# One core, attention recurrence, routing and experts: scans swapped, sat and m2 moved ahead, gate logits summed once from a table

## The chip, the cores and the metric

The kernel runs on one core of one Trainium2 chip. The metric is device time in microseconds (us), the median of the runs; lower is better.

## The reference

What is computed, cut to what matters:

```python
# r, k, v, w, a, b: [4, 8, 768, 40] float32
for t in range(768):                      # per batch and head, state is 40 x 40
    y[:, :, t] = einsum('bhd,bhde->bhe', rt, state)
    Sa = einsum('bhde,bhe->bhd', state, at)
    state = state * wt[:, :, None, :] - einsum('bhd,bhe->bhde', Sa, bt) + einsum('bhd,bhe->bhde', vt, kt)
x = y.transpose(0, 2, 1, 3).reshape(3072, 320)
# one expert of 8 per token: argmax and softmax of x @ w_gate
#   out[token] = gate * (relu(x @ w1[e]) @ w2[e])        w1 320 x 1024, w2 1024 x 320
# then a dense block: h = out @ w_in (320 x 2048); (max(h, 0) + alpha * min(h, 0)) @ w_out
```

## The kernel before

The program has three stages, one after the other: `attention` (with the routing at its end), `stage5_experts` and `stage6_dense`. The change is in `attention` alone.

`attention` cuts the 768 positions into 12 chunks of 64 and does 24 steps (`STEPS`), 16 of the 32 pairs of batch and head in each. Inside a chunk the recurrence is written as matrix products, so that only the 40 x 40 state goes from step to step. It has two passes over the steps.

**First pass**, 24 steps with no state in it. VectorE makes, for step j, the running products of the decay `w`: `suffixes(j)` scans backward (L437), `prefix_starts(j)` takes a reciprocal of the total (L442), `prefixes(j)` scans forward from it (L446). Then come two products of 512 columns, `scaled_second` (L453) and `scaled_alpha` (L456). TensorE multiplies these (`g1`, `bt`), ScalarE copies the results out of PSUM, and SyncE (SP) stores them to DRAM as blocks. The blocks are inverted on GpSimd (L118 to L127, eight steps on VectorE, L145 and L147) while the passes run on.

**Second pass**, the loop at L932 on TensorE, with a loop of its own on every other engine, 24 steps. All products of a step go through the helper `heads` (L784: 16 matmuls a product, which the trace counts as 32), in a fixed order, with a wait (`arrive`) ahead of each that needs a result of VectorE or ScalarE. Four double banks of PSUM are reused inside a step:

- BA: `alpha_s` and `g2_v` (done `w`), `low_part` (done `z`), `sat`, `m2`
- BB: `s`, then `m1` and in the end the sum that is done as `y`
- BC: `u`, `sa`, and `g2` of the next step
- BD: `ktm`, then the new state (done `st`), then `picks` (L846), which turns the rows of `yt` of the step before and multiplies them by the gate weights.

So `picks` waits for VectorE to have read the new state (`out_of["st"]`, the instruction that writes `swt` at L550), and the product that ends as `y` waits for VectorE's `m2` (L484, written from `m2_product`). VectorE does in this order in step k: `yt` of the step before (L461), its gate logits (`gates_of`, L466, read from PSUM), `alpha` for the next step (L456), the backward scan for the step after (L437), `m1` (L484), the reciprocal (L442), the sum into `w_tm` (L531), `second` (L453), the forward scan (L446), a copy of one column (L450), `swt` (L550), `m2` and `g2` (L484). ScalarE copies the products out of PSUM: `w_tm`, `st`, `ktm`, `sa_tm`, then `sa_tm` again (L758), `sat` (L760), the next inverse (L724) and the finished rows `picked` (L740). SP issues the loads, in order: the two halves of `wq` crossed between partitions (`cross_wq`), `t_in` three steps ahead, the store of `picked`, `vtm`, `vt`, an inverse, `rr`.

In the slots that are free in the last two steps VectorE does the first part of the routing (`choices_top`, L473 to L475, and `choices_one`, L479 and L480) for the 21 tiles of tokens whose logits are there by then. The last three tiles are done after the loop.

```python
                heads(from_b(lambda i, q, m: sa_tm[rows(m), slot(q ^ m, i), :]), BD, DIM, opens=False, done="st")
                arrive(out_of["sat"], i)
                heads(m2_product, BA, C, done="m2")
                arrive(s_second, i + (STEPS + 1))
                heads(with_alpha(second), BC, C, done="g2")
                arrive(out_of["st"], i + 1)
                picks()
                arrive(out_of["m2"], i)
                heads(from_b(lambda i, q, m: m2[rows(m), slot(q, i), :]), BB, C, opens=False, done="y")
```

## Time and profile before

| what | value |
| --- | --- |
| median of 3 runs | 1057.15 us (1055.74 to 1058.28) |
| profiled execution, its own time | 1054.7 us |
| its span, first to last instruction | 1052.9 us |
| TensorE matmul busy | 952.9 us (90%) |
| VectorE busy | 711.5 us (68%) |
| ScalarE busy | 442.8 us (42%) |
| GpSimd busy | 268.6 us (26%) |
| mean granted TensorE clock | 0.982 of full speed |

The span is what lies between the first and the last instruction of one execution; 1.8 us of its time lie around it. Busy shares are averages over stages that differ: the first pass runs from 0 to 139 us, the second from 139 to 373 us, the routing to 394 us, and the two expert stages fill the rest. PE is TensorE, PEld its weight loads, DVE VectorE, ACT ScalarE, POOL GpSimd, and a q behind a name is that engine's DMA queue.

### The profile page before, as it was taken

To read this page: it belongs to the slowest core of one execution; us is meant where nothing else is said; L and a number is where in the kernel's file an instruction comes from. 1 tells how busy PE (TensorE), PEld (TensorE's weight loads), DVE (VectorE), ACT (ScalarE), POOL (GpSimd) and SP (SyncE) were. 2 spreads that over 40 slices of the span, in tenths; PEclk is the share of its full clock that TensorE was granted. 3 is DMA by queue.
4 is the path that set the end of the run, shared out by engine and by line. 5 is a ranking of instruction groups with operands and counts; after the bars stand their busy time and mean duration, and the time that the engine had idled before them with its cause. 6 is when DMAs were issued, how large, how long until landed. Compare 5 with 4: busy or idle time off the path is not lost. (4 is left out here: it accounts for less than half of the span.)

```text
span 1052.9 us, 48691 instructions
## 1 busy us (share of the span) xinstructions
PE 952.9 (90%) x21425; PEld 874.8 (83%) x21425; DVE 711.5 (68%) x1076; ACT 442.8 (42%) x940; POOL 268.6 (26%) x348
## 2 busy tenths in 40 slices
PE   3526779999999998999999999879999999999997
PEld 2426769999999958998999999668999999999997
DVE  8997958899988764555555555567666565656664
ACT  5525635755555604545555555513222212222211
POOL 1009989798900003222111100241001000000000
PEclk9999988999999999999999999999999999999999
DMA  7968866898898539998676755120100101010100
GB/s 220 234 173 189 203 140 188 242 246 236 238 243 241 150 119 307 332 294 278 190 249 214 228 169 169 41 79 13 38 1 26 26 1 26 2 26 1 26 1 26
DMA packets 116866, 153.19 MB, mean 145 GB/s; under 512 B 68516, under 2 KB 87860, under 8 KB 116420
## 3 DMA queue, kind: packets, MB, share of 16 engines
q1 hardware_dynamic: 102468, 118.68, 40.3%
q0 software_dynamic: 5872, 25.28, 7.8%
q10 hardware_dynamic: 8464, 8.43, 2.4%
q8 instruction: 36, 0.59, 0.2%
q14 instruction: 26, 0.21, 0.1%
HBM read 126.72 MB, written 19.23 MB: 139 GB/s over the span
## 5 line engine op out<-in xcount | busy, mean ns | idle before, releaser
L1468 ACT CAST g_hi<-g 128x512 fp32r<-128x512 f32 x96 | 59.5, 620 | 278.0 <-DVE g L1412 274.4
L1321 PE MATMUL y_bank<-w_out_hi,g_hi 128*128 128x320 f32 x380 | 119.0, 313 | 5.1 <-DVE g_lo L1386 4.3
L1109 PE MATMUL h_bank<-xt,w 128*128 128x128 f32 x992 | 122.0, 282 | 1.8 <-issue 1.8
L1149 DVE TENSOR_TENSOR w_lo<-w_all,w_hi 128x640 fp32r<-128x640 f32 x124 | 101.7, 826 | 31.9 <-ACT w_hi L1189 27.0
L1109 PEld LDWEIGHTS h_bank<-xt,w 128*128 128x128 f32 x992 | 115.8, 195 | 6.0 <-issue 2.2
L1321 PE MATMUL y_bank<-w_out_hi,g_lo 128*128 128x320 f32 x380 | 118.0, 310 | 0.0
L1321 PE MATMUL y_bank<-w_out_lo,g_hi 128*128 128x320 f32 x380 | 117.9, 310 | 0.0
L1408 DVE TENSOR_SCALAR neg<-h_bank,slope 128x512 f32<-128x512 f32 x96 | 72.0, 750 | 65.8 <-PE h_bank L1308 65.4
L1308 PE MATMUL h_bank<-xt_hi,w_in_hi 128*128 128x512 f32 x288 | 113.1, 393 | 0.5 <-DVE xt_hi L1369 0.5
L1308 PE MATMUL h_bank<-xt_hi,w_in_lo 128*128 128x512 f32 x288 | 112.1, 389 | 0.0
L1386 DVE TENSOR_TENSOR g_lo<-g,g_hi 128x512 fp32r<-128x512 f32 x96 | 66.5, 693 | 65.9 <-ACT g_hi L1468 64.5
L1142 DVE SCALAR_TENSOR_TENSOR ht_lo<-h_bank,ht_hi 128x512 fp32r<-128x512 f32 x62 | 42.8, 692 | 88.6 <-ACT ht_hi L1182 83.7
L1189 ACT CAST w_hi<-w_all 128x640 fp32r x124 | 89.7, 727 | 29.3 <-PE y_bank L1121 20.6
L127 POOL TENSOR_TENSOR solved<-solved,share 128x31 f32<-128x31 f32 (+15 forms) x124 | 99.2, 800 | 9.7
L784 PE MATMUL bank<-alpha,second 40*64 40x64 f32 x1568 | 44.6, 269 | 56.5 <-DVE alpha L456 55.7
L124 POOL TENSOR_TENSOR share<-solved,blk 128x31 f32<-128x31 f32 (+15 forms) x124 | 89.0, 718 | 9.7
L784 PEld LDWEIGHTS bank<-alpha,second 40*64 40x64 f32 x1568 | 38.6, 178 | 59.8 <-issue 59.8
L95 POOL DMA_INDIRECT x<-x_rows_mid,order x31 | 32.1, 1035 | 197.8 <-DVE order L609 97.5
L1321 PEld LDWEIGHTS y_bank<-w_out_hi,g_hi 128*128 128x128 f32 x380 | 71.9, 189 | 10.6 <-DVE g_lo L1386 5.9
L1121 PE MATMUL y_bank<-w_hi,ht_hi 128*128 128x320 f32 x248 | 79.2, 319 | 0.0
L1182 ACT ACTIVATE ht_hi<-h_bank 128x512 fp32r<-128x512 f32 x62 | 37.1, 598 | 97.3 <-PE h_bank L1109 97.3
L1121 PE MATMUL y_bank<-w_lo,ht_hi 128*128 128x320 f32 x248 | 76.7, 309 | 0.0
(213 smaller groups left out, 2145.1 us busy)
## 6 DMA issues: line engine op xcount, KB each, us to landing
w<-w_in SPq DMA_DIRECT2D x31, 1024.0 KB
t_in<-wak_in SPq DMA_DIRECT2D x24, 679.0 KB, 5.7
t_in<-wab_in SPq DMA_DIRECT2D x21, 679.0 KB, 5.0
w_all<-w_in POOLq DMA_DIRECT2D x8, 1280.0 KB, 9.2
rr<-rr_in SPq DMA_DIRECT2D x24, 336.0 KB, 3.5
w_rest<-w_in SPq DMA_DIRECT2D x62, 128.0 KB
vtm<-vtm_in SPq DMA_DIRECT2D x24, 240.0 KB, 3.7
vt<-vt_in SPq DMA_DIRECT2D x24, 224.0 KB, 4.0
```

What stands on the lines that cost most here:

```text
L124: link(eng.tensor_tensor(part, q[:, 0:j + 1, j:j + 1].to_broadcast(shape), h[:, j:j + 1, j + 1:B].to_broadcast(shape), ALU.mult))
L127: link(eng.tensor_tensor(rest, rest, part, ALU.subtract))
L784: last = pe.matmul(out[HALF * to:HALF * to + rows_out, row, n * i:n * i + n], lhs, rhs, start=opens and i == 0, stop=closes and i == HP - 1)
L1109: last = pe.matmul(h_bank[s][h][:, f * ET:(f + 1) * ET], w1[s][:, k, (FH * h + f) * PARTS:(FH * h + f + 1) * PARTS], xt[s][:, k, :], start ...
L1121: last = pe.matmul(y_bank[s][:, 0:FEAT], h[s][:, f, :], w[:, f, :], start=f == 0 and n == 0, stop=f == NF - 1 and n == 2)
L1149: dve.tensor_tensor(piece(w2_lo, p), of_expert(e, p), piece(w2_hi, p).bitcast(F32), ALU.subtract).then_inc(s_w2lo, 1)
L1189: act.copy(piece(w2_hi, p), of_expert(e, p)).then_inc(s_w2hi, 1)
L1308: last = pe.matmul(h_bank[j % 2][:, :], w[:, k, f * PARTS:(f + 1) * PARTS], x_part[b % 2][:, k, :], start=n == 0, stop=n == len(passes) - 1)
L1321: last = pe.matmul(y_bank[n][:, 0:FEAT], g_part[j % RING][:, n * PARTS:(n + 1) * PARTS], v[:, f, :], start=f == 0 and p == 0, stop=f == NF ...
L1386: dve.tensor_tensor(g_lo[j % RING][:, :], g[j % 2][:, :], g_hi[j % RING][:, :].bitcast(F32), ALU.subtract).then_inc(s_glo, 1)
L1408: dve.tensor_scalar(neg[j % 2][:, :], h_bank[j % 2][:, :], 0.0, keep.slope[:, f:f + 1], ALU.min, ALU.mult).then_inc(s_neg, 1)
L1468: act.copy(g_hi[j % RING][:, :], g[j % 2][:, :]).then_inc(s_ghi, 1)
```

## The change

VectorE's two scans change places in both passes. The forward scan `prefixes` now comes first, the reciprocal (`suffix_starts`) is taken from its end, and the backward scan `suffixes` second. In the first pass `alpha` now comes ahead of `second`. The total decay that `swt` is multiplied by is now column C of the step's own `wq`, so the copy at L450 goes. SP's `cross_wq` waits for the forward scan of its step and, from its third call on, for the `yt` of two steps before (earlier: three steps before).

On TensorE `sat` now stands ahead of `sa`, and `m2` ahead of the product that ends as `st`. ScalarE copies `sat` ahead of `sa_tm`, and VectorE writes `m2` ahead of `swt`.

VectorE's reduce in each step of the second pass (`gates_of(k)`, 64 columns of PSUM to 8) goes. In its place ScalarE copies the 64 columns of a step into a table `gate_parts`, in memory of the first expert weights that is not in use yet, ahead of its copy of `picked`. VectorE sums 21 steps of the table in one reduce in the slot of step k = 22, ahead of `choices_top`, and the last three in one after the loop. TensorE's `ktm` waits for ScalarE's `picked` in place of VectorE's reduce.

```diff
+        gate_parts = keep.w1[0][:, :, :].rearrange("q n f -> q (n f)")[:, 0:STEPS * 2 * QP * EXPERTS].rearrange("q (k n) -> q k n", k=STEPS)
...
             def load_t(j):
                 if j >= TR:
-                    if j - TR < STEPS:
-                        sp.wait_ge(s_alpha1, j - TR + 1)
-                    elif j - TR == STEPS:
-                        sp.wait_ge(s_alpha0, 1)
-                    else:
-                        sp.wait_ge(s_second, j - TR + 1)
+                    sp.wait_ge(s_second, j - TR + 1)
...
             def cross_wq(k):
-                sp.wait_ge(s_wc, k + 1)
-                if k >= 3:
-                    sp.wait_ge(out_of["y"], k - 1)
+                sp.wait_ge(s_wq, STEPS + k + 1)
+                if k >= 2:
+                    sp.wait_ge(out_of["y"], k)
...
             def store_rows(k):
-                sp.wait_ge(s_rows, k + 1)
+                sp.wait_ge(s_rows, k + 3)
...
+            def prefixes(j):
+                dve.wait_ge(s_t[j % TR], 16 * (j // TR + 1))
+                if j >= 1:
+                    dve.wait_ge(s_suf, j)
+                dve.tensor_tensor_scan(out=forward(wq[j % 3][:, :, :]), data0=forward(w_of(j)), data1=forward(restart[:, :, :]), initial=0.0,
+                                       op0=ALU.mult, op1=ALU.add).then_inc(s_wq, 1)
+
+            def suffix_starts(j):
+                dve.wait_ge(s_wq, j + 1)
+                dve.reciprocal(restart[:, :, WIDE - 1:WIDE], wq[j % 3][:, :, C:C + 1]).then_inc(s_rw, 1)
+
             def suffixes(j):
-                dve.wait_ge(s_t[j % TR], 16 * (j // TR + 1))
+                dve.wait_ge(s_rw, j + 1)
                 if j >= 2:
                     dve.wait_ge(s_second, j - 1)
...
-            def prefix_starts(j):
+            def scaled_second(j):
                 dve.wait_ge(s_suf, j + 1)
-                dve.reciprocal(restart[:, :, 0:1], suf[j % 2][:, :, 1:2]).then_inc(s_rw, 1)
...
-            def prefixes(j):
-                dve.wait_ge(s_rw, j + 1)
...
-                dve.wait_ge(s_wq, j + 1)
-                if j >= STEPS:
-                    dve.tensor_copy(wq[j % 3][:, :, WIDE - 1:WIDE], suf[j % 2][:, :, 1:2]).then_inc(s_wc, 1)
...
-            def scaled_second(j):
...
-            def scaled_alpha(j, sem):
-                dve.tensor_tensor(alpha[:, :, :], in_of(j, 0), wq[j % 3][:, :, 0:C], ALU.mult).then_inc(sem, 1)
+            def scaled_alpha(j):
+                return dve.tensor_tensor(alpha[:, :, :], in_of(j, 0), wq[j % 3][:, :, 0:C], ALU.mult)
...
-            def gates_of(k):
-                dve.wait_ge(s_rows, k + 1)
-                gates = BD[:, :, 0:QP * PICK].rearrange("q h (p e) -> q e h p", e=PICK)[:, DIM:PICK]
-                dve.tensor_reduce(logit[:, k, :], gates, mybir.AxisListType.XY, ALU.add).then_inc(out_of["pick"], 1)
+            def gates_of(steps):
+                return dve.tensor_reduce(logit[:, steps, :], gate_parts[:, steps, :].rearrange("q k (x e) -> q k e x", e=EXPERTS), AX, ALU.add)
...
             for k in range(STEPS):
+                prefixes(k)
+                suffix_starts(k)
                 suffixes(k)
-                prefix_starts(k)
-                prefixes(k)
                 if k >= 1:
                     dve.wait_ge(did["bt"], k)
+                scaled_alpha(k)
                 scaled_second(k)
-                scaled_alpha(k, s_alpha1)
...
+            prefixes(STEPS)
+            suffix_starts(STEPS)
             suffixes(STEPS)
-            prefix_starts(STEPS)
-            prefixes(STEPS)
             dve.wait_ge(did["bt"], STEPS)
+            scaled_alpha(STEPS).then_inc(s_alpha0, 1)
             scaled_second(STEPS)
...
-            suffixes(STEPS + 1)
+            prefixes(STEPS + 1)
+            suffix_starts(STEPS + 1)
...
-            prefix_starts(STEPS + 1)
-            prefixes(STEPS + 1)
+            suffixes(STEPS + 1)
...
-                    if k >= 2:
-                        gates_of(k - 2)
-                    else:
-                        dve.sem_inc(out_of["pick"], 1)
                 dve.wait_ge(did["w"], k + 1)
                 if more:
-                    scaled_alpha(STEPS + k + 1, s_alpha)
+                    scaled_alpha(STEPS + k + 1).then_inc(s_alpha, 1)
                 if k + 2 < STEPS:
-                    suffixes(STEPS + k + 2)
+                    if k >= 1:
+                        dve.wait_ge(out_of["y"], k + 1)
+                    prefixes(STEPS + k + 2)
                 dve.wait_ge(did["m1"], k + 1)
                 masked(m1, BB).then_inc(out_of["m1"], 1)
                 if k + 2 < STEPS:
-                    prefix_starts(STEPS + k + 2)
+                    suffix_starts(STEPS + k + 2)
...
                 if k + 2 < STEPS:
-                    prefixes(STEPS + k + 2)
+                    suffixes(STEPS + k + 2)
                 elif k + 2 == STEPS:
                     dve.wait_ge(s_iota, 8)
+                    dve.wait_ge(s_gates, NTT - LATE)
+                    first_choices(gates_of(FIRST))
                     choices_top(FIRST, first_choices)
                 else:
                     dve.memset(one_hot[:, :, FINAL], 0.0)
                     choices_one(FIRST, first_choices).then_inc(s_hot, 1)
+                dve.wait_ge(did["m2"], k + 1)
+                masked(m2, BA).then_inc(out_of["m2"], 1)
                 dve.wait_ge(did["st"], k + 1)
                 if (k + 1) % NCHUNK == 0:
                     last = dve.memset(swt[:, :, :], 0.0)
                 else:
-                    dve.wait_ge(s_wqx[(k + 1) % 2], 32 * turn(k + 1))
+                    dve.wait_ge(s_wqx[k % 2], 32 * turn(k))
                     last = dve.tensor_tensor(by_row(swt), BD[:, :, 0:HP * DIM].rearrange("q r (p e) -> q r p e", e=DIM),
-                                             own_and_crossed(k + 1, slice(WIDE - 1, WIDE)).to_broadcast([PARTS, 2, HP, DIM]), ALU.mult)
+                                             own_and_crossed(k, slice(C, C + 1)).to_broadcast([PARTS, 2, HP, DIM]), ALU.mult)
                 last.then_inc(out_of["st"], 1)
-                dve.wait_ge(did["m2"], k + 1)
-                masked(m2, BA).then_inc(out_of["m2"], 1)
                 if more:
                     dve.wait_ge(did["g2"], k + 2)
...
-            gates_of(STEPS - 2)
...
-            gates_of(STEPS - 1)
-            dve.wait_ge(out_of["pick"], STEPS + 2)
+            dve.wait_ge(s_gates, STEPS)
+            link(gates_of(FINAL))
             choices_top(FINAL, link)
...
             def rows_of(k):
                 act.wait_ge(did["pick"], k + 2)
+                both = BD[:, :, 0:QP * PICK].rearrange("q h (p e) -> q h p e", p=QP)
+                act.copy(gate_parts[:, k, :].rearrange("q (h p e) -> q h p e", h=2, p=QP), both[:, :, :, DIM:PICK]).then_inc(s_gates, 1)
                 if k >= 2:
                     act.wait_ge(s_xst[k % 2], 16 * turn(k - 2))
-                act.copy(picked[k % 2][:, :].rearrange("q (p h e) -> q h p e", p=QP, h=2),
-                         BD[:, :, 0:QP * PICK].rearrange("q h (p e) -> q h p e", p=QP)[:, :, :, 0:DIM]).then_inc(s_rows, 1)
+                act.copy(picked[k % 2][:, :].rearrange("q (p h e) -> q h p e", p=QP, h=2), both[:, :, :, 0:DIM]).then_inc(s_rows, 1)
...
+                act.wait_ge(did["sat"], k + 1)
+                act.copy(by_row(sat[:, :, :]), wide(BA)).then_inc(out_of["sat"], 1)
                 act.wait_ge(did["sa"], k + 1)
                 act.copy(flat(sa_tm[:, :, :]), narrow(BC)).then_inc(out_of["sa"], 1)
-                act.wait_ge(did["sat"], k + 1)
-                act.copy(by_row(sat[:, :, :]), wide(BA)).then_inc(out_of["sat"], 1)
...
             def g1_product(count):
-                arrive(s_alpha1, count)
+                arrive(s_second, count)
...
+            pe.sem_inc(s_rows, 2)
...
-                arrive(out_of["pick"], i)
+                arrive(s_rows, i)
                 heads(turned(second), BD, DIM, done="ktm")
...
                 arrive(out_of["z"], i)
+                heads(sat_product, BA, C, done="sat")
                 heads(sa_product, BC, DIM, done="sa")
-                heads(sat_product, BA, C, done="sat")
                 heads(from_s(lambda i, q, m: at_m(rr, i, q, m, live(m))), BB, C, opens=False, closes=False)
+                arrive(out_of["sat"], i)
+                heads(m2_product, BA, C, done="m2")
                 arrive(out_of["sa"], i)
                 heads(from_b(lambda i, q, m: sa_tm[rows(m), slot(q ^ m, i), :]), BD, DIM, opens=False, done="st")
-                arrive(out_of["sat"], i)
-                heads(m2_product, BA, C, done="m2")
                 arrive(s_second, i + (STEPS + 1))
                 heads(with_alpha(second), BC, C, done="g2")
                 arrive(out_of["st"], i + 1)
```

On TensorE, in one step of the second pass, from the `m1` product to the `y` product (bank0 is BA, bank1 BB, bank2 BC, bank3 BD; `w_tm,inv` is `sa`, `inv,w_tm` is `sat`, `rr,sat` is `m2`, `sa_tm,btm` is `st`, `m2,btm` is `y`). Before:

```order
L784 MATMUL bank1<-m1,ktm 40x64 x16
L784 MATMUL bank2<-w_tm,inv 64x40 x16
L784 MATMUL bank0<-inv,w_tm 40x64 x16
L784 MATMUL bank1<-rr,st 40x64 x16
L784 MATMUL bank3<-sa_tm,btm 40x40 x16
L784 MATMUL bank0<-rr,sat 64x64 x16
```

The same place in the changed kernel:

```order
L778 MATMUL bank1<-m1,ktm 40x64 x16
L778 MATMUL bank0<-inv,w_tm 40x64 x16
L778 MATMUL bank2<-w_tm,inv 64x40 x16
L778 MATMUL bank1<-rr,st 40x64 x16
L778 MATMUL bank0<-rr,sat 64x64 x16
L778 MATMUL bank3<-sa_tm,btm 40x40 x16
```

`sat` and `sa` have changed places, and so have `m2` and `st`. Behind them stand in both kernels `g2`, `picks` and `y`, in this order.

On VectorE, in one step of the second pass, with what each instruction waits for (`pe_` is a product of TensorE that is done). Before:

```order
L456 TENSOR_TENSOR alpha<-t_in1,wq1 128x512 [waits pe_w]
L437 SCALAR_TENSOR_TENSOR suf0<-t_in2,restart 128x528 [waits s_second,s_t2]
L484 TENSOR_TENSOR m1<-bank1,later 128x512 [waits pe_m1]
L442 RECIPROCAL restart<-suf0 128x8 [waits s_suf]
L531 TENSOR_TENSOR w_tm<-w_tm,bank0 128x320 [waits pe_z]
L453 TENSOR_TENSOR second<-t_in1,suf1 128x512 [waits pe_ktm]
L446 SCALAR_TENSOR_TENSOR wq2<-t_in2,restart 128x528 [waits s_rw]
L450 COPY wq2<-suf0 128x8 [waits s_wq]
L550 TENSOR_TENSOR swt<-bank3,wq1 128x320 [waits s_wqx1,pe_st]
L484 TENSOR_TENSOR m2<-bank0,later 128x512 [waits pe_m2]
L484 TENSOR_TENSOR g2<-bank2,later 128x512 [waits pe_g2]
```

The same place in the changed kernel:

```order
L452 TENSOR_TENSOR alpha<-t_in1,wq1 128x512 [waits pe_w]
L433 SCALAR_TENSOR_TENSOR wq2<-t_in2,restart 128x528 [waits s_suf,s_t2]
L478 TENSOR_TENSOR m1<-bank1,later 128x512 [waits pe_m1]
L438 RECIPROCAL restart<-wq2 128x8 [waits s_wq]
L523 TENSOR_TENSOR w_tm<-w_tm,bank0 128x320 [waits pe_z]
L449 TENSOR_TENSOR second<-t_in1,suf1 128x512 [waits s_suf,pe_ktm]
L444 SCALAR_TENSOR_TENSOR suf0<-t_in2,restart 128x528 [waits s_second,s_rw]
L478 TENSOR_TENSOR m2<-bank0,later 128x512 [waits pe_m2]
L546 TENSOR_TENSOR swt<-bank3,wq0 128x320 [waits s_wqx0,pe_st]
L478 TENSOR_TENSOR g2<-bank2,later 128x512 [waits pe_g2]
```

The forward scan stands first, the copy is gone, and `m2` stands ahead of `swt`.

## Rows read from the trace of the kernel before

**Rows 1.** Stretches: us; busy of PE, PEld, DVE, ACT, POOL; clock; DMA share; GB/s.

```profile
139.00:170.00 31.00, 25.91 (x1173) 25.07 (x1173) 17.10 (x24) 12.69 (x33) 27.51 (x46) 0.67 0.50 130
170.00:291.00 121.00, 116.42 (x7483) 110.96 (x7475) 109.83 (x169) 75.03 (x189) 106.59 (x147) 1.00 0.89 239
291.00:373.00 82.00, 79.52 (x5200) 75.75 (x5189) 64.11 (x114) 46.22 (x113) 1.33 (x5) 1.00 0.74 200
```

**Rows 2.** Timeline, TensorE, one step with GpSimd idle: start, duration, instruction.

```profile
300.56 0.22 PE L784 MATMUL bank<-swt,alpha 40*64 40x40 f32 x1 [0.20 <-issue]
...
305.22 0.66 PE L784 MATMUL bank<-w_tm,inv 64*64 64x40 f32 x32
...
306.57 0.52 PE L784 MATMUL bank<-sa_tm,btm 64*40 64x40 f32 x32
307.12 0.69 PE L784 MATMUL bank<-rr,sat 40*64 40x64 f32 x32
...
308.08 0.66 PE L846 MATMUL bank<-pick,yt 40*64 40x48 f32 x32
308.71 0.66 PE L784 MATMUL bank<-m,btm 64*40 64x64 f32 x32
309.57 0.22 PE L784 MATMUL bank<-swt,alpha 40*64 40x40 f32 x1 [0.20 <-issue]
```

**Rows 3.** Timeline, ScalarE, the same step.

```profile
305.94 0.43 ACT L758 COPY sa_tm<-bank 128x320 f32<-128x320 f32 x1 [1.95 <-PE bank L784]
306.39 0.59 ACT L760 COPY sat<-bank 128x512 f32<-128x512 f32 x1
```

**Rows 4.** Timeline, VectorE, the same step.

```profile
305.58 1.25 DVE L446 TENSOR_TENSOR_SCAN wq<-t_in,restart 128x528 f32<-128x528 f32 x1
...
307.15 0.49 DVE L550 TENSOR_TENSOR swt<-bank,wq 128x320 f32<-128x320 f32 x1
307.88 0.69 DVE L484 TENSOR_TENSOR m<-bank,later 128x512 f32<-128x512 f32 x1 [0.24 <-PE bank L784]
308.49 0.68 DVE L484 TENSOR_TENSOR g<-bank,later 128x512 f32<-128x512 f32 x1
```

**Rows 5.** Timeline, VectorE, a step beside GpSimd's inversions.

```profile
268.39 1.78 DVE L446 TENSOR_TENSOR_SCAN wq<-t_in,restart 128x528 f32<-128x528 f32 x1
...
270.56 0.47 DVE L550 TENSOR_TENSOR swt<-bank,wq 128x320 f32<-128x320 f32 x1
270.96 0.67 DVE L484 TENSOR_TENSOR m<-bank,later 128x512 f32<-128x512 f32 x1
```

**Rows 6.** Timeline, TensorE, the end of that step.

```profile
271.18 0.68 PE L846 MATMUL bank<-pick,yt 40*64 40x48 f32 x32 [0.19 <-DVE swt L550]
271.78 0.66 PE L784 MATMUL bank<-m,btm 64*40 64x64 f32 x32
```

**Rows 7.** Timeline, VectorE, one step of the first pass, to its second instruction.

```profile
23.03 1.26 DVE L446 TENSOR_TENSOR_SCAN wq<-t_in,restart 128x528 f32<-128x528 f32 x1
24.32 0.69 DVE L453 TENSOR_TENSOR second<-t_in,suf 128x512 f32<-128x512 f32 x1
```

**Rows 8.** Timeline, VectorE, the routing in the slot of step k = 22.

```profile
360.15 0.32 DVE L473 TENSOR_REDUCE top<-logit 128x21 f32<-128x168 f32 x1
...
361.11 0.34 DVE L475 TENSOR_TENSOR late<-late,descend 128x168 f32<-128x168 f32 x1
```

**Rows 9.** Timeline, VectorE, reduces of 192 elements, strided input, then contiguous.

```profile
381.27 0.62 DVE L597 TENSOR_REDUCE total<-late 128x24 f32<-128x192 f32 x1
...
389.13 0.34 DVE L612 TENSOR_REDUCE top<-late 128x24 f32<-128x192 f32 x1
```

**Rows 10.** Timeline, SP's queue, the same step as rows 2.

```profile
300.92 0.59 SPq L282 DMA_DIRECT2D t_in<-wak_in  x1
...
304.56 0.35 SPq L332 DMA_DIRECT2D vtm<-vtm_in  x1
```

**Rows 11.** One line of the kernel, L332 (the load of `vtm`), 130 to 372 us.

```profile
DMA to landing us min/median/max: 2.6/3.7/5.0
```

19 lines of the change are left out of this document (8 added, 11 removed).

## The prediction

> **What bounds the kernel now.** I read the busy time by stretches first. The expert stages are not touched, so only the first 394 us count. In the second pass TensorE is busy nearly all the time: 116.4 of 121 us while GpSimd inverts, 79.5 of 82 us after that [rows 1]. A step of `heads` is 18 products of 32 counted matmuls, 576, so these stretches hold 13 steps (7483) and 9 (5200), and the one before them 2 (1173) [rows 1]. A busy TensorE says little here, because the ends of its matmuls are modelled. So next I read the timeline of one clean step.
>
> A clean step takes 9.01 us, from 300.56 to 309.57 [rows 2]. Its last part is a chain with no slack. I give times from the step's start, 300.56. The product in the place of `sa` starts at 4.66 [rows 2]; ScalarE copies `sa_tm` at 5.38 and `sat` at 5.83, to 6.42 [rows 3]; `m2` starts at 6.56, although TensorE was through with the 0.35 us or so of `st`, begun at 6.01, before that [rows 2]; VectorE writes `m2` from 7.32 to 8.01 after a wait of 0.24 us for TensorE [rows 4]; the `y` product starts at 8.15, and the next step 0.86 us later [rows 2]. `picks` starts at 7.52 and doesn't wait, because `swt`, which it needs, ended at 7.08 [rows 2, 4]. VectorE waits for TensorE here, so taking work off VectorE is worth nothing in such a step.
>
> A step beside GpSimd is another matter: VectorE's scan takes 1.78 us in place of 1.25, and scan, copy, `swt` and `m2` follow one another with no gap [rows 4, 5]. `picks` waits for `swt` and `y` for `m2` [rows 6]. Here VectorE sets the pace. That step takes about 9.85 us (262.79 to 272.63 between the starts of its first products, an estimate from the same view); the mean over the 13 steps is 121/13 = 9.3.
>
> **First pass: the swapped scans, alpha ahead of second.** Today `second` waits for the scan just ahead of it: the scan starts at 23.03, ends at 24.29, and `second` starts at 24.32, 1.29 us after it [rows 7]. In the new order `alpha` stands behind the second scan and doesn't need it, and `second` comes after `alpha`. An instruction that waits for nothing starts before the one ahead has ended: `g2` 0.61 us after `m2`, which takes 0.69 [rows 4]. So the scan's slot becomes 1.26 - 0.08 = 1.18 us, a gain of 0.11 us in each of 24 steps: **-2.6 us**. Where VectorE waits for TensorE or a DMA it is nothing; the ends are -2.6 and 0. TensorE's `g1` waits for the last of the two products as before, and SP's load of `t_in` too.
>
> The Trainium skill, "VectorE: DVE Perf Modes", section "The DRAIN you can't avoid", speaks against this: the pipe empties after each operation, and a semaphore between two costs nothing more. By it this term would be 0 and the sum 2.6 us higher. Rows 4 disagree, since `g2` starts 0.08 us before `m2` ends, and so the sum goes by the rows.
>
> **Second pass, clean step.** `sat` now takes the slot that starts at 4.66, so ScalarE copies it from 5.38 to 5.97 instead of 5.83 to 6.42. `m2` can start 0.14 us after that (6.56 against 6.42), at 6.11, which is also when `rr,st` is through. VectorE's `m2` follows 0.76 us behind (7.32 against 6.56), at 6.87. So far this is 0.45 us ahead of today. But `swt` now stands behind `m2`: it starts 0.61 us later at 7.48, takes 0.49, ends at 7.97. `st` is done by then (it starts at 6.59, and `swt` could start 0.58 us behind it). `picks` needs `swt` and starts 0.15 us later, at 8.11 (271.18 against 271.03 in rows 5, 6), where today it starts at 7.52. `y` needs `m2` only, but it stands behind `picks` in TensorE's order, whose 32 matmuls take 0.47 us to issue (an estimate: those of `st` to `m2` apart, the groups of rows 2 follow each other in 0.45 to 0.49). So `y` starts at 8.58 instead of 8.15: **+0.43 us a clean step**. What was side by side, `picks` beside VectorE's `m2`, is now in a row. The copy at L450 and the logit reduce that go were hidden in VectorE's waits and give nothing here.
>
> **Second pass, step beside GpSimd.** Today `y` starts 1.61 us behind the end of the scan: 271.78 against 268.39 + 1.78 = 270.17 [rows 5, 6]. In the new order `m2` starts 0.08 us before the scan's end (or when TensorE has it), `swt` 0.60 later, ends after 0.48, `picks` 0.15 later, `y` 0.47 later: 1.62 us. The 0.39 us of the copy, from 270.17 to 270.56 [rows 5], pay for the 0.47 us of `picks`. So such a step stays the same. Between the two kinds I interpolate by length: at the mean of 9.3 us, (9.85 - 9.3)/(9.85 - 9.01) = 0.65 of 0.43, that is 0.28; with the later steps nearer the slow end I take 0.25, times 13: **+3.2 us**.
>
> **The other steps.** Two steps lie in the stretch with the clock at 0.67 of full speed, that is partly at the lower of its two levels, 1.2 GHz [rows 1]. There matmuls take twice as long, `picks` among them: 0.43 to 0.8 a step, **+1.1 us**. Of the last 9 steps 8 are clean: **+3.4 us**.
>
> **Step k = 22.** Its slot on VectorE now begins with the reduce of 21 steps: 21 x 64 = 1344 elements, 32 bytes apart. The rows have 192 elements in 0.34 us when contiguous and 0.62 us when strided [rows 9]. 168 contiguous ones take 0.32 [rows 8], so each further one costs 0.02/24, about 1 ns, and a strided one (0.62 - 0.34)/192 = 1.46 ns more. From 0.34 us at 1 ns for 1152 further elements the lower bound is 1.5 us; from 0.62 at 2.46 ns the upper is 3.45. I take the upper, since the input is strided. Then the 1.30 us of the routing follow, from 360.15 to 361.45 today [rows 8], and `m2`, `swt`, `picks`, `y` behind them in a row: the slot starts at 5.02, where the scan stands in a clean step [rows 4], so 5.02 + 3.45 + 0.04 + 1.30 - 0.08 = 9.73, and `y` 0.61 + 0.49 + 0.15 + 0.47 later at 11.45 against 8.15: **+3.3 us** (with the lower bound +1.4). Today's 1.30 us are hidden; the cover is gone because the slot has only 1.8 us (5.02 to 6.87).
>
> The Trainium skill, "SBUF — State Buffer", section "Door 1: The DMA port swizzle", says that an fp32 operand strides for free up to 4 elements, and here the step is 8, against 24 in the strided row. If short strides were free the sum would be 1.9 us lower.
>
> **After the loop.** The last three steps are reduced from the table, 192 strided elements at 0.62 us [rows 9] in place of 64 of PSUM, and ScalarE copies the small part first: **+0.2 us** (0 to +0.5).
>
> **DMA.** SP's crossing of `wq` now waits for the last `yt`, which ends 0.55 us into the next step, and `t_in` stands behind it: with 1.1 us for the two issues it goes out at about 1.7 us instead of 0.36 [rows 10]. `vtm` is issued at 4.00 and lands 3.7 us later, 5.0 at most [rows 10, 11]. If it is pushed back by the full 1.35 us it lands at 9.05, against a need at about 9.2 in a step of 9.44. The engines are at 0.89 of their time [rows 1]. I take 0, with -1 (waits of today that the longer step hides) and +6 as ends (0.3 us in each of some 20 steps).
>
> **The sum.** -2.6 + 3.2 + 1.1 + 3.4 + 3.3 + 0.2 = +8.6 us. The profiled execution took 1054.7 us, so 1063.3 by its own measure. It lies 2.45 us under the median of 1057.15, and against that the forecast is **1066 us**. A change of 0.2%, about 2.1 us, is what a measurement of this kernel can tell from none.
>
> **Rivals.**
> 1. *Chain shortened, faster.* `m2` is on VectorE 0.45 us earlier. If the work of VectorE sets the pace of most steps (109.8 of 121 us busy, rows 1), the copy's 0.39 us and the reduce's slot go straight into time: 13 x -0.39 = -5.1, -2.6 in the first pass, and if `picks` doesn't hold `y` in the others -0.2 x 9: about -9, 1048 us. It decides where `swt` ends early enough for `picks` at 7.52, that is by 7.37; from a start of `m2` at 6.87 only 0.50 us are left for 1.10 us of work. Against it. Chance 0.11.
> 2. *It cancels.* GpSimd's neighbours behave as the slow step (13 x 0), the big reduce costs 1.4 and the half-speed steps nothing: -2.6 + 3.4 + 1.4 = +2, or less: 1057 to 1059. Chance 0.09.
> 3. *The queue.* The later `t_in` pushes `vtm` and `rr` past their need in most steps: +6 on the forecast, 1072; more is braked, since a late step start brings `yt` nearer to it. Chance 0.12.
> 4. Forecast, with 1060 to 1071 as its own range. Chance 0.68.
>
> Faster 0.11, same 0.09, slower 0.80. The range goes from 1057.5, the middle of rival 2, to 1074.
>
> **What would show it.** In a clean step: `m2` on VectorE at 6.9 us, `swt` behind it at 7.5, `picks` with an idle of some 0.6 us ended by `swt`, `y` 0.47 us behind `picks`, a period of 9.44. Slow steps at 9.8. First pass: 3.92 us a step instead of 4.03. The reduce at L460 at 3.4 us. I am wrong if `picks` isn't held by `swt`, if `y` waits for `m2`, or if the period is under 9.1.

## The result, and the profile after

The changed kernel took **1071.83 us** (median of 4 runs, 1067.3 to 1076.26) against 1056.45 for the kernel before in the same comparison: 1.0153 times as long, 95% interval 1.0118 to 1.0189. On a second chip the same pair gave 1.0117 (1.007 to 1.0163). It is slower, by 15.4 us between the medians here and by 12.2 on the second chip. Its profiled execution took 1067.3 us with a span of 1065.5, and is the lowest of the four. The ratios here and below leave out executions more than 1.5% above the fastest of their kernel, which are three of 12 in `a_undo_order`, four of 12 in `a_sum_spread`, one of 12 in `b_scans` and one of the 23 of the kernel before on the second chip; with all of them the ratios of the means would be 1.0083, 1.0101 and 1.0061.

The busy times from the page of the changed kernel:

```profile
PE 954.4 (90%) x21425; PEld 877.6 (82%) x21425; DVE 703.0 (66%) x1030; ACT 443.2 (42%) x964; POOL 266.8 (25%) x348
```

VectorE is busy 8.5 us less and TensorE 1.5 us more, and yet the end is 12.6 us later. So most of the loss is time in which TensorE stands idle. The stretches that answer to [rows 1], in the same columns:

```profile
138.00:168.00 30.00, 26.01 (x1176) 24.95 (x1172) 16.62 (x22) 12.69 (x34) 26.89 (x41) 0.66 0.53 140
168.00:296.00 128.00, 116.40 (x7510) 110.89 (x7502) 103.85 (x144) 75.22 (x203) 107.72 (x152) 1.00 0.92 225
296.00:375.00 79.00, 70.85 (x4591) 67.46 (x4583) 59.04 (x88) 42.53 (x112) 0.00 (x0) 1.00 0.82 205
```

The 13 steps beside GpSimd fill 128 us instead of 121 with the same 116.4 us of TensorE. The last row has only 8 steps (4591 matmuls) in 79 us, where the kernel before has 9 in 82. I cut the way to stage 5 at the starts of the first product of a step, as in [rows 2], and at the stage's first transpose:

| part, us | before | changed | difference |
| --- | --- | --- | --- |
| start of the second pass | 139.04 | 137.77 | -1.3 |
| steps 0 and 1 | 30.68 | 29.85 | -0.8 |
| steps 2 to 21 | 185.37 | 195.95 | +10.6 |
| step 22 | 9.05 | 11.68 | +2.6 |
| step 23 and what follows, to stage 5 | 29.75 | 34.24 | +4.5 |
| stages 5 and 6, to the end | 659.0 | 656.0 | -3.0 |

**A clean step** (against [rows 2]), TensorE's timeline of the changed kernel; start, duration, instruction:

```profile
305.22 0.22 PE L778 MATMUL bank<-swt,alpha 40*64 40x40 f32 x1 [0.35 <-issue]
...
311.33 0.69 PE L778 MATMUL bank<-rr,sat 40*64 40x64 f32 x32
311.82 0.52 PE L778 MATMUL bank<-sa_tm,btm 64*40 64x40 f32 x32
312.26 0.69 PE L778 MATMUL bank<-alpha,second 40*64 40x64 f32 x32
313.32 0.68 PE L840 MATMUL bank<-pick,yt 40*64 40x48 f32 x32 [0.36 <-DVE swt L546]
313.79 0.66 PE L778 MATMUL bank<-m,btm 64*40 64x64 f32 x32
314.80 0.22 PE L778 MATMUL bank<-swt,alpha 40*64 40x40 f32 x1 [0.34 <-DMA vtm<-vtm_in]
```

and VectorE's in it (against [rows 4]):

```profile
312.08 0.69 DVE L478 TENSOR_TENSOR m<-bank,later 128x512 f32<-128x512 f32 x1 [0.58 <-PE bank L778]
312.69 0.48 DVE L546 TENSOR_TENSOR swt<-bank,wq 128x320 f32<-128x320 f32 x1
```

`m2` (`rr,sat`) starts 6.11 us into the step, VectorE writes it from 6.86, `swt` follows at 7.47, `picks` waits for `swt` and starts at 8.10, `y` at 8.57. The next step begins 1.01 us behind `y`, and not 0.86 as in [rows 2]. Its idle time of 0.34 us is put down to the load of `vtm`, but in steps in which nothing is late it is 0.30 us as well.

**Step 22**, VectorE; the first row is the reduce of the table:

```profile
368.59 2.63 DVE L460 TENSOR_REDUCE logit<-w 128x168 f32<-128x1344 f32 x1
371.25 0.33 DVE L467 TENSOR_REDUCE top<-logit 128x21 f32<-128x168 f32 x1
...
372.59 0.69 DVE L478 TENSOR_TENSOR m<-bank,later 128x512 f32<-128x512 f32 x1
373.20 0.48 DVE L546 TENSOR_TENSOR swt<-bank,wq 128x320 f32<-128x320 f32 x1
```

and TensorE from there into **step 23**:

```profile
373.82 0.68 PE L840 MATMUL bank<-pick,yt 40*64 40x48 f32 x32 [2.53 <-DVE swt L546]
...
376.10 1.10 PE L778 MATMUL bank<-vtm,g 64*64 64x40 f32 x32
...
383.21 1.08 PE L778 MATMUL bank<-inv,w_tm 64*40 64x64 f32 x32
```

TensorE waited 2.53 us for `swt`. From 375.1 us on, for 10.2 us, its granted clock was 0.5 of full speed, the lower level of 1.2 GHz ("half clock" below): a product's start is 0.85 us behind the last one's instead of 0.46.

**The transfers.** SP's queue in the clean step (against [rows 10]), one of the worst waits for `rr`, and the groups of the loads of `vtm` (against [rows 11]):

```profile
305.70 1.11 SPq L341 DMA_DIRECT2D wq<-wq  x2
306.86 0.59 SPq L278 DMA_DIRECT2D t_in<-wak_in  x1
...
309.24 0.35 SPq L328 DMA_DIRECT2D vtm<-vtm_in  x1
...
312.08 0.33 SPq L323 DMA_DIRECT2D rr<-rr_in  x1
```

```profile
180.59 0.69 PE L778 MATMUL bank<-rr,vt 40*64 40x64 f32 x32 [0.98 <-DMA rr<-rr_in]
```

```profile
who waited for it (us, times):
  PE bank L778: 2.4, 6
...
DMA to landing us min/median/max: 2.7/4.9/5.7
```

`t_in` goes out 1.64 us into the step, behind the crossing, and `vtm` takes 4.9 us to land instead of 3.7 (medians). The product of `rr` and `vt`, at 2.34 us of a step when nothing is late, starts later in many: summed over the 20 middle steps (2 to 21) 4.3 us of lateness, 0.7 before. Where a number of steps with a late `rr` is given below, it is those with more than 0.3 us.

### The profile page after: what moved, and what is told of

Its sections match the earlier page's. It is cut to its first block and busy times, and to the rows that moved or that the text cites. A ratio compares the mean times of both kernels' runs of the same rounds, so it can differ in the third digit from the quotient of the medians.

```text
span 1065.5 us, 48696 instructions
## 1 busy us (share of the span) xinstructions
PE 954.4 (90%) x21425; PEld 877.6 (82%) x21425; DVE 703.0 (66%) x1030; ACT 443.2 (42%) x964; POOL 266.8 (25%) x348
## 5 line engine op out<-in xcount | busy, mean ns | idle before, releaser
L1381 DVE TENSOR_TENSOR g_lo<-g,g_hi 128x512 fp32r<-128x512 f32 x96 | 66.5, 693 | 65.9 <-ACT g_hi L1463 64.5
L127 POOL TENSOR_TENSOR solved<-solved,share 128x31 f32<-128x31 f32 (+15 forms) x124 | 94.7, 764 | 9.7
L124 POOL TENSOR_TENSOR share<-solved,blk 128x31 f32<-128x31 f32 (+15 forms) x124 | 93.5, 754 | 9.7
```

The source lines that it names most:

```text
L124: link(eng.tensor_tensor(part, q[:, 0:j + 1, j:j + 1].to_broadcast(shape), h[:, j:j + 1, j + 1:B].to_broadcast(shape), ALU.mult))
L127: link(eng.tensor_tensor(rest, rest, part, ALU.subtract))
L1381: dve.tensor_tensor(g_lo[j % RING][:, :], g[j % 2][:, :], g_hi[j % RING][:, :].bitcast(F32), ALU.subtract).then_inc(s_glo, 1)
```

## The experiments

For each I give the timed ratio to the kernel before, and from one trace the row of exactly steps 2 to 21 (first product to first product; columns as in [rows 1]): its second number is the length. The two kernels themselves give, over two traces each, 185.36 and 185.69 us before, 195.96 and 194.66 changed.

```profile
169.71:355.07 185.36, 178.58 (x11520) 170.09 (x11521) 164.13 (x261) 112.56 (x281) 108.13 (x152) 1.00 0.88 237
```

```profile
167.62:363.58 195.96, 178.78 (x11521) 170.29 (x11521) 154.89 (x221) 112.91 (x302) 108.10 (x152) 1.00 0.91 224
```

**1. The order alone** (`b_order`): the kernel before with

```diff
-                heads(sa_product, BC, DIM, done="sa")
                 heads(sat_product, BA, C, done="sat")
+                heads(sa_product, BC, DIM, done="sa")
...
-                arrive(out_of["sa"], i)
-                heads(from_b(lambda i, q, m: sa_tm[rows(m), slot(q ^ m, i), :]), BD, DIM, opens=False, done="st")
                 arrive(out_of["sat"], i)
                 heads(m2_product, BA, C, done="m2")
+                arrive(out_of["sa"], i)
+                heads(from_b(lambda i, q, m: sa_tm[rows(m), slot(q ^ m, i), :]), BD, DIM, opens=False, done="st")
```

and the same exchange on ScalarE and VectorE.

> The kernel before with the new order of products alone: `sat` ahead of `sa`, `m2` ahead of `st` and of `swt`; scans, gates and SP's queue as before. Theory (`picks` is held by `swt`, which stands behind `m2` on VectorE, and the time from `picks` to the next step is 1.48 us whether `y` waits or not): a clean step has `m2` on VectorE at 6.87, `picks` at 8.1, `y` at 8.57 and a period of 9.5 to 9.57 instead of 9.01; steps beside GpSimd are as long as before or 0.2 longer; no late `rr` (product of `rr` and `vt` at 2.34 to 2.5) and no half clock in step 23; 20 middle steps 6 to 9 us longer, 1.006 to 1.009 of the kernel before. Rival (it is the late queue and not the order that made the changed kernel's steps long): periods of 9.0 to 9.1 in the clean steps, 0.999 to 1.002.

1.0116 (1.007 to 1.0162), and

```profile
168.05:362.28 194.23, 178.13 (x11520) 170.47 (x11521) 161.50 (x261) 110.23 (x280) 108.09 (x154) 1.00 0.82 225
```

Clean steps take 9.50 us, `rr` is never late, step 23 keeps its clock. The order by itself costs 8.7 us in these steps, nearly the changed kernel's whole loss there (9.8 on the mean of its two traces), with no late transfer. The timed ratio can't be told from the changed kernel's 1.0117 on the same chip. And the order costs as much beside GpSimd, where I expected 0 to 0.2 us a step (127.7 us for 13 steps, 121.9 before, the mean of two traces; 0.45 a step) as in clean ones (66.5 for 7, 63.6 before; 0.41). VectorE in one of the slow ones:

```profile
202.58 1.63 DVE L446 TENSOR_TENSOR_SCAN wq<-t_in,restart 128x528 f32<-128x528 f32 x1
204.25 0.41 DVE L450 COPY wq<-suf 128x8 f32<-128x8 f32 x1
204.57 0.68 DVE L484 TENSOR_TENSOR m<-bank,later 128x512 f32<-128x512 f32 x1
205.17 0.47 DVE L552 TENSOR_TENSOR swt<-bank,wq 128x320 f32<-128x320 f32 x1
```

`picks` and `y` follow `swt`, with the copy still in the chain ahead.

**2. The scans alone** (`b_scans`): the kernel before with the swapped scans, `alpha` first, no copy at L450, and the later crossing

```diff
             def cross_wq(k):
-                sp.wait_ge(s_wc, k + 1)
-                if k >= 3:
-                    sp.wait_ge(out_of["y"], k - 1)
+                sp.wait_ge(s_wq, STEPS + k + 1)
+                if k >= 2:
+                    sp.wait_ge(out_of["y"], k)
```

> The kernel before, with the two scans swapped alone: `alpha` ahead of `second`, the copy at L450 gone, the crossing of `wq` behind `yt`; the order of products and the gates are as before. If my accounts of the parts add up: first pass 1.3 us shorter as in the changed kernel (137.8 instead of 139.0 us at the start of the second pass), middle steps longer by the late `t_in` alone, 3 to 4 us, and no slow step 23: time +2 to +3 us, 1.002 to 1.003. Rival (in the steps beside GpSimd the copy's 0.39 us were on the chain, and there is nothing now to take their place): 13 steps are 0.2 to 0.39 us shorter, 2.6 to 5.1 us, which pays for the transfers; 0.996 to 1.000.

1.0045 (1.0011 to 1.0079), and

```profile
167.52:363.80 196.28, 181.44 (x11523) 172.76 (x11524) 159.65 (x241) 113.47 (x281) 106.31 (x152) 0.97 0.90 224
```

Neither: 10.8 us more in the 20 steps, where I expected 3 to 4. `rr` is late in 11 steps, 7.2 us in all. `vtm` is late too: the step after begins more than 0.86 us behind `y`, by 5.0 us in all. And one step of 13.09 us ran mostly at half clock, behind

```profile
284.30 0.22 PE L782 MATMUL bank<-swt,alpha 40*64 40x40 f32 x1 [1.62 <-DMA vtm<-vtm_in]
```

So the scans, with the crossing that goes with them, cost by themselves about as much in these steps as the order does, and the two together not the sum of both. The timed loss is only 4.7 us, and this trace's execution (1059.3 us) is at the median. Outside the 20 steps it is shorter than those of the kernel before: the second pass begins 2.0 us sooner, and stages 5 and 6 take 654.9 us against 659.0 and 661.3, which goes with the clock there (see the bullet on these stages below).

**3. The order undone in the changed kernel** (`a_undo_order`), the reverse of the diff of 1.

> The changed kernel, with the order of `sa`/`sat`, `st`/`m2` and `swt`/`m2` as before; scans, gate table and the queue's order stay as changed. Theory 1 (in the changed kernel `picks` is held by `swt` behind `m2`, and `y` by `picks`: the trace has `picks` at 8.10 and `y` at 8.57 of a clean step, 8.15 before, and the next step 1.00 us after `y` instead of 0.86): `picks` is back at 7.5 and `y` at 8.15 of a clean step, the next step 0.86 us behind it, and the 20 middle steps take 0.43 to 0.57 us less in the clean ones and up to 0.2 less beside GpSimd, 5 to 8 us in all; time about 0.5 to 0.7% below the changed kernel's 1.015 of the kernel before, 1.008 to 1.010. Rival (the late transfers of `rr` and `vtm` set the step anyway, the order only fills their wait): `rr` and `vtm` are still late, the more so because a shorter step needs them earlier, and less than 3 us come back, 1.013 or more. Rival from the slot: the reduce of the gates in step 22 and the half-clock step behind it stay as they are, some 7 us, under either theory.

1.0069 (1.0031 to 1.0107), and

```profile
167.20:361.44 194.24, 180.41 (x11521) 171.66 (x11521) 156.73 (x221) 115.89 (x303) 107.52 (x152) 0.98 0.91 226
```

In this trace about 1 us comes back in the 20 steps, as the rival has it, and the timed ratio lies on theory 1's side (the profiled execution took 1068.5 us, the median is 1065.7). So this run doesn't decide between them by itself. The steps in which everything arrives in time are 9.0 to 9.5 us long again (`picks` at 7.51, 9.01 in step 21), so theory 1 is right about the chain. But `rr` is now late in 9 steps, 7.0 us in all, and behind two of its waits, of 1.02 and 1.47 us, TensorE fell to half clock for 3.4 us. The second:

```profile
221.04 0.69 PE L778 MATMUL bank<-rr,vt 40*64 40x64 f32 x32 [1.47 <-DMA rr<-rr_in]
```

**4. `t_in` first** (`a_tin_first`):

```diff
             for k in range(STEPS):
                 more = k + 1 < STEPS
-                if more:
-                    cross_wq(k + 1)
                 if k + TR < STEPS:
                     load_t(STEPS + k + TR)
+                if more:
+                    cross_wq(k + 1)
```

> The changed kernel, but SP issues the loads of `t_in` ahead of the crossing of `wq`, so that they don't stand behind its wait for the last `yt`; the crossing itself still waits. Theory (the late queue makes `rr` late: the product of `rr` and `vt` starts 0.2 to 1.1 us behind its usual place of 2.34 in most steps, some 4.3 us over 20 steps against 0.7 before): the product is back at 2.34 to 2.5, `vtm` lands no later than before, and the 20 middle steps are 3 to 4 us shorter; 1.011 to 1.012 of the kernel before. Rival (it is the crossing's own lateness, or the engines' load, and not `t_in`): no more than 1 us comes back, 1.014 to 1.015. Second rival (the crossing, now later by the issue of `t_in`, holds `yt` or `swt`, which read it): `swt` and `yt` on VectorE wait for it and the steps grow; 1.016 or more.

1.0136 (1.0089 to 1.0184), and

```profile
167.46:360.02 192.56, 178.26 (x11521) 170.38 (x11521) 154.56 (x221) 112.60 (x301) 108.81 (x153) 1.00 0.85 227
```

The product of `rr` and `vt` starts at 2.34 in all 20 steps, `vtm` lands in 2.8 us (median), and the 20 steps are 2.1 and 3.4 us shorter than in the changed kernel's two traces. The times alone can't show so small a gain. The edits of experiments 5 and 6 leave the order of products and SP's queue in these steps as in the changed kernel, so their traces are two more to compare with: 195.8 us and, with a half-clock stretch behind a wait of 1.24 us for `rr`, 198.4:

```profile
167.22:363.03 195.81, 178.88 (x11520) 170.38 (x11521) 157.76 (x241) 112.56 (x300) 108.07 (x154) 1.00 0.91 224
```

```profile
166.80:365.17 198.37, 180.15 (x11520) 171.80 (x11521) 154.62 (x221) 112.77 (x301) 107.32 (x154) 0.99 0.89 221
```

**5. The sum spread** (`a_sum_spread`):

```diff
                     y_out(k - 1)
+                    if k >= 2:
+                        dve.wait_ge(s_gates, k - 1)
+                        first_choices(gates_of(slice(k - 2, k - 1)))
...
-                    dve.wait_ge(s_gates, NTT - LATE)
-                    first_choices(gates_of(FIRST))
                     choices_top(FIRST, first_choices)
...
-            link(gates_of(FINAL))
+            link(gates_of(slice(NTT - 2, NTT)))
```

> The changed kernel, but VectorE sums the table one step at a time, behind `yt`, and the last two steps after the loop; nothing else differs. Theory (the one large reduce costs twice: 2.6 us in step 22, where the trace has it from 5.02 on, and about 4.5 us in step 23, which runs at a granted clock of 0.5 behind TensorE's idle time): step 22 takes about 9.6 us instead of 11.68, step 23's `y` starts near 8.6 instead of 12.64, at full clock, and the kernel is 6 to 7 us faster than the changed one, 1.009 of the kernel before. Rival 1 (the half clock of step 23 has nothing to do with the reduce and comes anyway): only 2 to 2.6 us, 1.013. Rival 2 (the 22 small reduces stand ahead of `alpha` and the scan, and VectorE sets the pace of the 13 steps beside GpSimd): these steps grow by 0.2 to 0.3 us each, 2.6 to 3.9 us, and half of the gain goes.

1.007 (1.0028 to 1.0112). Steps 22 and 23, with two stretches of the trace:

```profile
363.00:372.60 9.60, 8.84 (x576) 8.50 (x577) 6.19 (x13) 5.32 (x14) 0.00 (x0) 1.00 0.45 131
372.60:382.00 9.40, 9.08 (x578) 8.77 (x579) 3.84 (x10) 3.53 (x9) 0.00 (x0) 1.00 0.05 17
```

Step 22 takes 9.58 us instead of 11.68, step 23 has its full clock, and the 20 steps before are as long as in the changed kernel (195.8), so the 22 small reduces are free. The large reduce cost 2.1 us, and the clock behind it 2.6 more by this trace (31.66 us from step 23 to stage 5 against 34.24). What is left there against 29.75 before goes with a half-clock stretch of 6.8 us in the routing, where the kernel before has one of 3.4.

**6. The table without gaps** (`a_contig`):

```diff
-                act.copy(gate_parts[:, k, :].rearrange("q (h p e) -> q h p e", h=2, p=QP), both[:, :, :, DIM:PICK])
+                act.copy(gate_parts[:, k, :].rearrange("q (e h p) -> q h p e", h=2, p=QP), both[:, :, :, DIM:PICK])
...
-                gate_parts[:, steps, :].rearrange("q k (x e) -> q k e x", e=EXPERTS)
+                gate_parts[:, steps, :].rearrange("q k (e x) -> q k e x", e=EXPERTS)
```

> The changed kernel, but ScalarE writes a step's gate parts with the eight parts of one expert side by side, so that VectorE's reduce of 21 steps reads its 1344 elements without gaps; ScalarE's copy writes with the stride instead. If the stride of 32 bytes is what costs (my bounds were 1.5 us contiguous and 3.45 strided, and the trace had 2.63): the reduce takes 1.5 to 1.6 us, step 22 takes 10.6 us instead of 11.68, and step 23 may keep its full clock, 1 to 5 us less in all. If a stride of 8 fp32 costs nothing and a reduce of this size simply takes 2.6: 2.6 us again, and everything else as in the changed kernel. ScalarE's copy ahead of `picked` stays at its time, or grows by up to 0.2 us, which its waits hide.

```profile
370.20 1.55 DVE L460 TENSOR_REDUCE logit<-w 128x168 f32<-128x1344 f32 x1
```

1.55 us instead of 2.63, and step 22 takes 10.59. TensorE's wait is 1.1 us shorter, but step 23 runs at a granted clock of 0.5 all the same, now behind a wait of 1.45 us. 1.0108 (1.0075 to 1.0142).

**7. All three undone** (`c_best`, and `c_again`, the same kernel): what is left are the swapped scans and ScalarE's table.

> The changed kernel with all three undone at once: order of products as before, table summed one step at a time, `t_in` ahead of the crossing. What is left of the change is the swapped scans and ScalarE's table. Theory (the parts add up: the first pass keeps its gain, the rest of the loss is these three): start of the second pass 136 to 137.8 us instead of 139.0, clean steps 9.0, steps 22 and 23 9.0 to 9.1 at full clock, product of `rr` and `vt` at 2.34; steps beside GpSimd up to 0.39 us shorter, because VectorE's copy ahead of `m2` is gone: 0.993 to 0.998 of the kernel before. Rival (the crossing still waits for the last `yt` and lands later than before, and `swt` or `yt` wait for it; or ScalarE's extra copy ahead of `picked` delays the rows): steps 0.1 to 0.3 us longer, 1.000 to 1.005.

> The kernel of c_best once more: order of products as before, table summed a step at a time, `t_in` ahead of the crossing. In its first trace steps 5 and 6 took 9.99 and 13.73 us, because `rr` landed 0.8 and 2.0 us behind the usual start of its product and TensorE then ran at a granted clock of 0.5 for 6.8 us; the other 18 middle steps took 164.25 us, 9.13 each. If that was a chance meeting of transfers, this trace has no such step, the 20 middle steps take 182 to 184 us (185.4 before), and the time is 0.995 to 0.998 of the kernel before. If it is the rule with this queue's order, it is here again, in some step, and the time is 0.998 to 1.002.

0.9981 (0.9944 to 1.0017) and 0.9987 (0.9958 to 1.0015): no difference from the kernel before that could be measured. The two traces:

```profile
169.00:356.98 187.98, 179.62 (x11522) 171.51 (x11522) 158.00 (x241) 116.05 (x302) 106.43 (x150) 0.98 0.86 233
```

```profile
163.28:348.36 185.08, 177.00 (x11521) 168.81 (x11522) 160.13 (x241) 116.64 (x304) 114.24 (x157) 1.00 0.89 237
```

The steps in which nothing is late are as in the theory, 9.01 to 9.4 us. But `rr` was late in 2 and 3 of 20 steps (2.9 and 2.3 us in all), so it is no chance meeting. In the first trace one such wait, of 1.87 us, brought a step of 13.73 us with 6.8 us at half clock:

```profile
210.57 0.69 PE L779 MATMUL bank<-rr,vt 40*64 40x64 f32 x32 [1.87 <-DMA rr<-rr_in]
```

**8. `t_in` in the middle** (`c_tin_mid`): in that kernel, the issue of `t_in` moved behind `inv_in`.

> c_best, but SP issues `t_in`, the largest load (679 KB), behind `vtm`, `vt` and `inv_in`, about 5 us into the step, instead of ahead of the crossing at its end. Theory (what makes `rr` late is how much is queued on the DMA engines ahead of it, and `t_in` ahead of it is the worst): `rr`, issued 2 us behind `t_in`, lands later than in c_best, its product starts at 2.6 or later in most steps, some steps fall to half clock, and the 20 middle steps take 190 us or more, 1.004 or more of the kernel before. Rival (it is only the later issue of `vtm` behind the crossing's wait that hurts, and that stays out here as in c_best): as c_best, 0.995 to 1.000.

1.0401 (1.0363 to 1.0438), 40 us:

```profile
167.83:395.60 227.77, 198.92 (x11524) 190.30 (x11524) 159.59 (x241) 116.43 (x304) 101.91 (x152) 0.88 0.73 193
```

and the group of the loads of `rr` in it:

```profile
who waited for it (us, times):
  PE bank L779: 21.9, 13
```

Against `c_best` nothing but the place of one load has moved. The row's window ends at 372 us; over all 20 steps TensorE waits 23.7 us for `rr`, in 14 steps. Its clock is at half for 54 us of them, and most of the rest goes with that.

**9. `picks` last** (`d_picks_last`): order as changed, sum spread, `t_in` first, VectorE's `yt` waiting for `picks` of the step before as well, and

```diff
-                arrive(out_of["st"], i + 1)
-                picks()
                 arrive(out_of["m2"], i)
                 heads(from_b(lambda i, q, m: m2[rows(m), slot(q, i), :]), BB, C, opens=False, done="y")
+                arrive(out_of["st"], i + 1)
+                picks()
```

> The changed kernel with its order kept, but `picks` stands behind the `y` product on TensorE, the table is summed one step at a time and `t_in` goes ahead of the crossing. Theory (only `picks` needs `swt`; `y` needs `m2`, which is early): in a clean step `y` starts at 7.6 to 7.7 and `picks` at 8.11 behind `swt`, as the last product, and the next step 0.86 us behind it, a period of 8.97 to 9.0 against 9.50 with `t_in` first alone; `yt` may be formed 0.5 us earlier in its step. 0.993 to 0.998 of the kernel before, about as c_best. Rival (what follows `picks` sets the pace, not `picks`: ScalarE's two copies of the rows and the store, 0.47 us nearer to the next step's use of the same bank): the next step's product in that bank waits for ScalarE, period 9.3 or more, 1.003 or more.

0.9983 (0.9952 to 1.0013), and 186.61 us for the 20 steps. Clean steps take 9.08 instead of the 9.50 of `a_tin_first`, with one product moved, and `y` starts at 7.68 us instead of 8.55: it was `picks` that held it. It doesn't beat the old order: steps beside GpSimd take 9.46 us, 9.37 before. The next step begins 0.95 us behind `picks`, not the 0.86 that I expected.

**10. Both kernels again** (`before_again`, `after_again`).

> The kernel before once more, for a second trace of it: how much of the differences is chance. The start of the second pass at 138.5 to 139.5 us (the traces with the swapped scans have 135.6 to 137.8, the one with the old scans and the new order 138.7), clean steps 9.01, the 20 middle steps 184 to 187 us, `rr` late by less than 1 us in all, no half clock between the first two steps and the end of the second pass. If the first trace's 20 steps were luck, they take 189 us or more here, and the changed kernel's loss in them is smaller than I count.

> The changed kernel once more, beside the others on one chip, so that their differences have a common measure, and for a second look at its trace. If what I read in the first trace is structure: second pass begins at 136 to 138 us, clean steps 9.57, step 22 takes 11.7 us and step 23 runs at a granted clock of 0.5; the product of `rr` and `vt` is late by 3 to 6 us in all over the 20 middle steps, though not in the same ones. If step 23's clock or the lateness were chance, one of the two would be missing here. Ratio to the kernel before 1.012 to 1.019.

Both repeat what I read: 185.69 and 194.66 us for the 20 steps, 9.01 and 9.54 for a clean one, 11.68 for step 22, half clock in step 23 for 10.2 us, `rr` late by 0.2 and 3.3 us. One thing doesn't repeat: steps 0 and 1 took 24.5 us in this trace of the kernel before, 30.7 in the other. Over all 14 traces they take 24.5 to 31.8, with the number of half-clock stretches there, whatever the kernel. A gain or loss can't be read from them.

## Why the prediction was right or wrong

The forecast was 1066 with a range of 1057.5 to 1074; the time is 1071.8, and 1066.5 on the second chip. The sign and the cause named first hold: `picks` waits for `swt` behind `m2`, and `y` for `picks`. The number was in the range in part by luck. Two terms that I put at nothing, the clock in step 23 and the transfers, measure 7.2 us together, nearly as much as the whole sum of 8.6. And 1071.8 is rival 3's number without being rival 3's mechanism: the late transfers cost 2.1 to 3.4 us and not 6. Term by term:

- **First pass, -2.6.** The step goes from 4.03 to 3.89 us, though only in the first 15 or so. The later ones take 4.0 to 10 us in both kernels, so the gain isn't one of 24 steps. In the changed kernel VectorE's rows are

```profile
22.36 1.26 DVE L444 TENSOR_TENSOR_SCAN suf<-t_in,restart 128x528 f32<-128x528 f32 x1
23.54 0.67 DVE L452 TENSOR_TENSOR alpha<-t_in,wq 128x512 f32<-128x512 f32 x1
```

  with 1.18 us from scan to product, as worked out, 0.08 before the scan's end. The rule that gave 0 here, from the Trainium skill, "VectorE: DVE Perf Modes", section "The DRAIN you can't avoid", is not what these rows show. The section's first paragraph says itself that an operation that isn't held starts earlier, and I had left that out. The second pass starts at 136.7 us on the mean of the 11 traces with swapped scans, 138.9 on that of the 3 without: -2.2.
- **Clean step, +0.43.** Right row by row up to `y` (8.57 against 8.58), though `picks` idles 0.36 us and not 0.6; the period is 9.50 to 9.57, not 9.44. What failed is "the next step 0.86 us later", which I carried over. In the kernel before `y` waits for VectorE; where it doesn't wait, the next step starts 0.95 to 1.01 us behind it. Some 2 to 3 us over 20 steps. That the end of TensorE's loop is hidden behind a wait of `y` in the one and not in the other is my reading, and wasn't tried by itself.
- **Steps beside GpSimd, taken together +3.2.** `t_in` first, where the transfers are out of it, has 125.9 us for these 13 against 121.9: +4.0. The reason given, that the copy pays for `picks`, is borne out by `b_order`, which keeps the copy and loses 5.8.
- **Half-clock steps, +1.1.** Can't be told from chance (above).
- **Late clean steps, +3.4 for 8.** Seven took +3.0 with `t_in` first.
- **k = 22, +3.3.** +2.6. The mis-sized term is the reduce: 3.45 us taken, 2.63 measured. The lower bound of 1.5 is what it costs without gaps (1.55). My price of a strided element, 1.46 ns above a contiguous one, came from a row with steps of 24 elements. With steps of 8 it is (2.63 - 1.55)/1344 = 0.80 ns. That it isn't 0 is of a piece with the Trainium skill, "SBUF — State Buffer", section "Door 1: The DMA port swizzle", whose free stride ends at 4.
- **After the loop, +0.2.** The reduce took 0.50 us, not 0.62; the term is too small to be told from the next one.
- **Step 23, not in the sum.** +4.5: I priced TensorE's longer wait in step 22 at its own length only, and not the clock behind it.
- **DMA, 0 taken, -1 to +6.** "Lands at 9.05" came out: `vtm` is issued at 4.1 us and lands 4.9 us later (medians of the 20 steps). What failed is that I looked at `vtm` alone and left out `rr`. It is issued at 6.86 us and needed 5.1 us later, at 2.34 of the next step, and its product starts late by 4.3 us in all. Of the 2.4 us of waits put down to `vtm`, about 0.3 us in each of the six is there without it. Lateness costs 2.1 to 3.4 us by these two traces. Rival 3 is in part what happens.
- **Stages 5 and 6** take 3.0 and 3.3 us less than before in the two pairs of traces, though nothing in them was changed. That goes with the clock and not with the change, as far as the traces show: over all 14 they take 654.9 us (`b_scans`) to 663.0 (`d_picks_last`), on the whole the longer, the lower TensorE's mean granted clock there (0.997 and 0.984 for these two). That clock is 0.989 and 0.986 in the kernel before, 0.991 and 0.990 in the changed one.

The terms as measured, -2.2 + 7.0 (order and loop's end, by `a_tin_first`) + 2.8 (transfers) + 2.6 + 4.4, come to +14.6. The profiled pairs differ by 12.6 and 18.1, and without steps 0 and 1 and without stages 5 and 6, whose differences follow the clock there, by 16.4 and 14.2. The medians differ by 15.4 and 12.2.

What I would have got wrong with the right number is the claim that the terms add. In the 20 steps the order alone costs 8.7 us (`b_order`). The scans and the held queue with the old order cost 10.8 (`b_scans`) and 8.7 (`a_undo_order`). Both together cost 9.1 to 12.8 in four traces (the changed kernel's two and those of experiments 5 and 6), and not 17 to 20. In a step of 9.01 us a crossing that holds `t_in` makes `rr` late by 7.0 to 7.2 us in all; in one of 9.5 by 3.3 to 4.8. So the longer chain covers part of the late transfers, and undoing one part (experiments 3 and 4) brought back little. How much of each trace's number is chance stays open: three of the seven have half-clock stretches in these steps, and the order alone was traced once.

## What to carry to other kernels

Before a consumer is moved ahead, ask which later instruction stands behind the one that was pushed back: here the product that only needed `m2` stood in line behind one that needed `swt`, and moving that one product gave nearly the whole step back (9.08 us against 9.01). When two parts of a change each fill the other's waiting time, undo them together before judging either. And a wait in a TensorE loop can cost a multiple of its own length, because the clock may fall behind it, so one large piece of work in a single step is worth spreading over all steps even if its sum is the same.

## What was unexpected of the hardware

- Where the clock fell. In steps 2 to 23 TensorE's granted clock went to 0.5 behind gaps of 1.02, 1.24, 1.45, 1.47, 1.62, 1.87, 1.91 and 2.53 us. It didn't behind gaps of 0.94, 0.96 and 0.98, nor behind one of 1.09 in `b_scans` and one of 1.86 in `c_tin_mid`, where eight others of 1.78 to 2.62 brought it down. A middle step with such a stretch takes 11.5 to 15.9 us instead of 9.0 to 9.6, so such a gap costs more than itself.
- One load's place in a queue, with the DMA engines at 0.86 to 0.89 of their time (`c_best`, `c_again`), was worth 40 us of 1054.
- A next loop pass began 0.95 to 1.01 us behind its last product's start where that product hadn't waited, 0.86 to 0.90 where it had.
